# Moving attention blocks between partition quarters: quarters paired 0 with 1 instead of 0 with 2, in another issue order

## The reference

```python
scores = scale * np.matmul(q, k.transpose(0, 1, 3, 2))
thresh = np.max(scores, axis=-1, keepdims=True) - tau
scores = np.where(scores >= thresh, scores, -1000000000.0)
attn = softmax(scores)                      # exp, divided by the sum + 1e-9
x = np.matmul(attn, v)                      # to (2304, 512), heads side by side
h = x @ w_in                                # 512 -> 2048
x = (np.maximum(h, 0.0) + alpha * np.minimum(h, 0.0)) @ w_out
x = ((x @ w1) * (x @ w2)) @ w3 @ w_out2     # 512 -> 1024 -> 1024 -> 512
```

## Time and profile before

| | |
|---|---|
| median of 3 runs | 1023.04 us (1022.2 to 1023.9) |
| the profiled execution | 1022.2 us |
| its span, first to last instruction | 1020.1 us |
| mean granted TensorE clock | 0.987 |
| PE busy / PEld busy / DVE busy | 94% / 85% / 65% of the span |
| DMA moved | 146.95 MB, mean 144 GB/s |
| DMA moves `zbuf<-ybuf` | 256, of which 192 by SP and 64 by ACT |

### The profile page before, as it was taken

One profiled execution on the slowest core, in us unless ns is written; L12 is line 12 of the kernel. 1 busy time (PEld: TensorE's weight loads), 2 busy tenths in 40 slices (PEclk: granted clock), 3 DMA queues, 4 the chain that ended last, 5 costly groups with the idle time before them and its releaser, 6 DMA issues.

```text
span 1020.1 us, 18286 instructions
## 1 busy us (share of the span) xinstructions
PE 959.8 (94%) x6656; PEld 871.2 (85%) x6656; DVE 665.7 (65%) x1648; ACT 417.2 (41%) x976; POOL 514.7 (50%) x604
## 2 busy tenths in 40 slices
PE   3699967999999999999999999999999999999998
PEld 2566635787878787879999999999999999999998
DVE  6899998998999998932333242333765656657544
ACT  5666666666666666533323222222411212103111
POOL 4977878756666766432443333242732524426322
PEclk9799997999999999999999999999999999999999
DMA  7289898776868676657154222222150200200001
GB/s 270 74 256 283 264 323 234 218 211 205 239 188 250 176 217 200 194 158 292 71 191 160 93 94 93 92 94 75 49 207 1 94 1 1 94 1 21 28 1 47
DMA packets 57017, 146.95 MB, mean 144 GB/s; under 512 B 8544, under 2 KB 24928, under 8 KB 54880
## 3 DMA queue, kind: packets, MB, share of 16 engines
q1 hardware_dynamic: 45936, 113.35, 34.5%
q10 hardware_dynamic: 10992, 32.45, 10.9%
HBM read 74.33 MB, written 27.79 MB: 100 GB/s over the span
## 4 chain that ended last, share of the span: by engine, by line
PE 69%; DVE 13%; POOL 5%; issue 4%; DMA 4%; ACT 3%; SPq 1%; ACTq 1%; POOLq 0%
PE psum L843 18%; PE psum L802 11%; PE psum L788 10%; PE psum L855 10%; PE psum L747 9%; PE psum L709 6%; DVE nmx L1107 4%; PE psum L692 3%; DVE e_ring L1120 3%; PE psum L760 2%; DMA zbuf<-ybuf 2%; POOL g L1326 2%; DVE g_raw L1152 1%; DMA k_raw<-k 1%; POOL w_a L1326 1%
## 5 line engine op out<-in xcount | busy, mean ns | idle before, releaser
L1326 POOL TENSOR_TENSOR g<-g_raw,g 128x288 fp32r<-128x288 f32 x160 | 132.7, 840 | 227.5 <-ACT g L982 211.2
L692 PE MATMUL psum<-ks,qs 128*128 128x288 f32 x640 | 119.3, 315 | 39.6 <-DVE e_ring L1120 27.0
L692 PEld LDWEIGHTS psum<-ks,qs 128*128 128x128 f32 x640 | 99.4, 201 | 54.8 <-DVE e_ring L1120 36.7
L1355 POOL TENSOR_SCALAR e_ring<-e_ring,rden,uni 128x576 f32<-128x576 f32 x144 | 119.1, 828 | 53.6 <-DVE rden L1131 47.5
L944 ACT ACTIVATE e_ring<-psum,nmx 128x576 f32<-128x576 f32 x144 | 106.9, 742 | 81.8 <-DVE nmx L1107 81.8
L1152 DVE SCALAR_TENSOR_TENSOR g_raw<-g_raw,beta_sb,psum 128x288 f32<-128x288 f32 x128 | 65.3, 513 | 105.3 <-ACT g_raw L978 105.2
L978 ACT ACTIVATE g_raw<-psum 128x288 f32<-128x288 f32 x128 | 52.6, 411 | 167.8 <-PE psum L788 159.5
L1107 DVE TENSOR_REDUCE nmx<-psum 128x1 f32<-128x576 f32 x144 | 108.4, 753 | 17.9 <-PE psum L692 17.5
L1120 DVE SCALAR_TENSOR_TENSOR e_ring<-psum,thr,e_ring 128x576 f32<-128x576 f32 x144 | 115.3, 800 | 4.9 <-ACT e_ring L944 4.2
L1139 DVE STREAM_TRANSPOSE ybuf<-e_ring 128x576 f32<-128x576 f32 x144 | 110.6, 768 | 0.8 <-POOL e_ring L1355 0.8
L802 PE MATMUL psum<-g,w_b 128*128 128x288 f32 x768 | 106.0, 296 | 4.5 <-POOL g L1326 4.1
(11 more groups left out here) (86 smaller groups left out, 1410.0 us busy)
## 6 DMA issues: line engine op xcount, KB each, us to landing
zbuf<-ybuf SPq DMA_DIRECT2D x96, 180.0 KB, 3.8
zbuf<-ybuf SPq DMA_DIRECT2D x96, 144.0 KB, 3.9
xy<-xs SPq DMA_DIRECT2D x12, 1152.0 KB, 5.2
raw_a<-weights SPq DMA_DIRECT2D x49, 256.0 KB, 6.5
q_raw<-q ACTq DMA_DIRECT2D x16, 576.0 KB, 6.0
xs<-x_hl SPq DMA_DIRECT2D x32, 288.0 KB, 6.5
k_raw<-k ACTq DMA_DIRECT2D x15, 576.0 KB, 7.3
zbuf<-ybuf ACTq DMA_DIRECT2D x32, 180.0 KB, 4.9
```

Source lines behind the costliest of these rows:

```text
L692: last = mm(dst, qs[:, par, at:at + P], ks[:, par, part, h, cols], start=(m == 0), stop=(m == 2 * len(terms) - 1))
L1326: sub = lambda out_, a, hi: nc.gpsimd.tensor_tensor(out_, a, hi.bitcast(F32), ALU.subtract)
L1355: nc.gpsimd.tensor_scalar(e, e, rden[:, i:i + 1], uni[:, i:i + 1], ALU.mult, ALU.add)\
```

## The change

Group 0 now has source quarters 0 and 1, group 1 has 2 and 3. The rest tile has head 0's 64 rows in quarters 0 and 1 and head 1's in 2 and 3, so its two parts in `qs` are contiguous runs of 64 columns with one run of 128 zero columns between them, one memset for each buffer. The value products read neighbouring places of `zbuf`, and `x_half` writes neighbouring places of `x_hl`. The number and sizes of the moves, who issues them, in which steps, and what they wait for stay. Their order is new:

| | SP, in order of issue | ACT |
|---|---|---|
| before, y = 0 | (0,0) (2,2) (0,1) (2,3) (0,2) (2,0) | (0,3) (2,1) |
| before, y = 1 | (1,0) (3,2) (1,1) (3,3) (1,2) (3,0) | (1,3) (3,1) |
| after, y = 0 | (0,0) (0,1) (1,3) (0,2) (0,3) (1,0) | (1,1) (1,2) |
| after, y = 1 | (2,2) (2,3) (3,1) (2,0) (2,1) (3,2) | (3,3) (3,0) |

```diff
-SP_MOVES = [(0, 0), (1, 2), (0, 1), (1, 3), (0, 2), (1, 0)]
-ACT_MOVES = [(0, 3), (1, 1)]
...
-            return zbuf[:, y:QD:2, kt, at:at + (MAIN + (y == h)) * SQ]
+            return zbuf[:, 2 * y:2 * y + 2, kt, at:at + (MAIN + (y == h)) * SQ]
...
-        def shared_q(par):
-
-            return qs[:, par, 2 * MAIN * P:].rearrange("p (h a z i) -> p h a z i", h=2, a=2, z=2)
...
-            return shared_q(par)[:, h, :, h, :], q_raw[:, h, MAIN * P:].rearrange("p (a i) -> p a i", a=2)
+            at = 2 * MAIN * P + 3 * REST * h
+            return qs[:, par, at:at + REST], q_raw[:, h, MAIN * P:]
...
-            dst = [x_hl[:, par, hl, 0:MAIN * P].rearrange("p (t a i) -> p t a i", t=MAIN, a=QD)[:, :, y:QD:2, :]
+            dst = [x_hl[:, par, hl, 0:MAIN * P].rearrange("p (t a i) -> p t a i", t=MAIN, a=QD)[:, :, 2 * y:2 * y + 2, :]
...
-                for b, c in SP_MOVES:
-                    sp.dma_start(*move(n, y, b, c)).then_inc(s_z[y], 16)
+                for k in range(QD):
+                    dst, src = move(n, 2 * y, (2 * y + k) % QD)
+                    sp.dma_start(dst, src).then_inc(s_z[y], 16)
+                    if k % 2 == 1:
+                        dst, src = move(n, 2 * y + 1, (2 * y + 3 + k // 2) % QD)
+                        sp.dma_start(dst, src).then_inc(s_z[y], 16)
...
-                act.dma_start(*move(n, y, *ACT_MOVES[half])).then_inc(s_z[y], 16)
+                dst, src = move(n, 2 * y + 1, (2 * y + 1 + half) % QD)
+                act.dma_start(dst, src).then_inc(s_z[y], 16)
...
-                for h in range(2):
-                    nc.vector.memset(shared_q(par)[:, h, :, 1 - h, :].bitcast(F32), 0.0)
+                nc.vector.memset(qs[:, par, 2 * MAIN * P + REST:2 * MAIN * P + 3 * REST].bitcast(F32), 0.0)
```

More of the change, by code:

```diff
@@ L440, in lo_part @@
                 return ks[:, n % 2, 1, part, cols], raw[:, cols], hi[:, cols]
-            if low >= 8:
-                return hi[DH:P, :, :], raw[DH:P, :, :], hi[DH:P, :, :]
-            cols = slice(low % 2 * 2 * P, (low % 2 + 1) * 2 * P)
+            cols = slice(low % 2 * 2 * P, (low % 2 + 1) * 2 * P) if low < 8 else slice(0, REST)
             return hi[DH:P, cols], raw[DH:P, cols], hi[DH:P, cols]
@@ L461, in x_piece, with move @@
             return x_rest(n % 2, part // 2) if part % 2 else x_half(n % 2, part // 2)
-        def move(n, y, b, c):
-            a = y + 2 * b
+        def move(n, a, c):
             return (zbuf[c * SQ:(c + 1) * SQ, a, 0:FIRST[c + 1] - FIRST[c], :],
```

## The result

| | before | after |
|---|---|---|
| median (8 runs each, same chip) | 1023.07 us | 1035.96 us |
| lowest to highest | 1022.04 to 1024.78 | 1029.22 to 1039.43 |
| profiled span | 1020.1 us | 1035.7 us |

The ratio is 1.0124, with a 95% interval of 1.0094 to 1.0152: slower by 12.9 us. Run a second time, beside other kernels, it was 1.0107 (1.0065 to 1.0150). The forecast was 1026.1 us in a range of 1021.0 to 1033.0: the right sign, a quarter of the size, and the range misses. The profiled execution of after is one of the longer ones, so its stretches add up to more than the median difference.

What follows compares the result with a forecast made beforehand. PE was taken as the bound, with DMA engines nearly full in pairs 3 and 4. Pairs 0 to 4 2.8, pair 12 0.6, ACT's smaller move -0.3: 3.1 us, from 1023.04 to 1026.1 us, range 1021.0 to 1033.0.

Steps and rivals of the forecast that it cites:

- What bounds the kernel; which waits are tight: PE bounds most pairs, DMA engines nearly full in 3 and 4; ten groups of pairs 0 to 4 have at most 0.31 us.
- The 20 us read from the moves' 2% of the chain: Whole kernel: 2% of 1020.1 us, taken as all the path time the change can reach through the moves.
- Layout and memsets at 0: Copies, memsets, PE's weight loads and value products: the new layout was taken to cost or save 0 us.
- The rate of a burst in one half: SP's six moves of a group: 251 to 207 GB/s, costing 0 to 0.84 us a group; 0.28 us taken.
- In pairs 0 to 2 PE has nothing to hide it.: Pairs 0 to 2: both groups' later landings, 2 x 0.28 = 0.56 us a pair, reach PE in full.
- the rival of the separated queues: Pairs 0 to 4: ACT's second move lands earlier, giving 1020 to 1021 us; chance 0.11 over 2 us faster, 0.03 less.
- In pairs 3 and 4 ... I take it in full: Pairs 3 and 4: DMA engines lack room, delayed weight loads make PE wait; 0.56 us a pair charged in full.
- the signs that I had named for being wrong: Earlier group 0 landings, weight loads of pair 3 or 4 shifting beyond the moves' own time, or a moved low-clock stretch.
- Later pairs, 0.6 us: After pair 4 only pair 12 has no slack, +0.6 us; slack covers pairs 6, 8 and 10.
- My upper end for the sum, 1035.6 us: Whole kernel at 0.84 us a group: 8.4 for pairs 0 to 4, 1.7 and 2.8 later, less 0.3: 12.6 us.

Runs made afterwards that it cites:

- e15: The kernel after, unchanged, measured a second time beside other kernels: 1035.29 us, ratio 1.0107 to before.
- e2: The kernel after with source quarters 1 and 2 exchanged, so that each group reads both halves: 1024.91 us, ratio 1.0012 to before.
- e7: The kernel after with the order of before inside each group: 1029.72 us, ratio 1.0057 to before.
- e10: The kernel after with SP's sources alternating between the group's two quarters and destinations in two runs of three in one half: 1039.73 us, ratio 1.0141 to before.
- e18: The kernel after with half of the key and query loads for pairs 8 to 15 alone: 1034.71 us, ratio 1.0102 to before.
- e5: The kernel before with half of the key and query loads from pair 1 on: 1021.20 us, ratio 0.9961 to before.
- e6: The kernel after with half of the key and query loads from pair 1 on: 1024.37 us, ratio 1.0000 to before.
- e17: The kernel before with half of the key and query loads for pairs 1 to 7: 1020.48 us, ratio 0.9962 to before.

## Why the prediction was wrong

*What bounds the kernel; which waits are tight.* Held: PE, and pairs 3 and 4 near-full. That the ten groups of pairs 0 to 4 land just ahead of PE was read rightly, but PE did not wait longer at each of them: in pair 2 it waited 0.59 us before and not at all after. The 20 us read from the moves' 2% of the chain were no bound, since a chain can grow: after, its page gives the moves 4% and SP's issuing of them (L526) another 4%. Groups with slack before became waits: group 1 of pairs 6, 10 and 12, pair 14 besides, pair 8 not; in e15 it is pairs 8, 10, 12 and 14. Two of them, after:

```profile
233.49 0.20 PEld L702 LDWEIGHTS psum<-zbuf,vs 128*64 128x64 f32 x4 [0.71 <-DMA zbuf<-ybuf]
...
396.93 0.20 PEld L702 LDWEIGHTS psum<-zbuf,vs 128*64 128x64 f32 x4 [1.44 <-DMA zbuf<-ybuf]
```

*Layout and memsets at 0.* Held: e2 and e7, and the durations at equal clock.

*The rate of a burst in one half.* The bounds, 251 and 207 GB/s, held; the choice of a third between them was too small. The burst ran at 219 GB/s: 995/219 = 4.54 us for six moves, 0.57 us more than 3.97, where I took 0.28. The Trainium skill, in SBUF — State Buffer, section "Door 1: The DMA port swizzle", gives about 218 GB/s for one half of the partitions, and this case's traces agree, with 213 to 222 in the first burst of the twelve kernels that read one half. The same page, section "Can I just issue two DMAs to hit both halves?", has only 6% for two DMAs on different halves over a single one. That is not quite this case, and a queue of alternating moves gains more here: 255 against 219 GB/s is 16%. I took a small value because in pairs 0 to 4 packets of loads stand between those of the moves. By e2, e7 and e10 that reasoning has no support: amid the loads even the order within a half costs time, and the rate of the lone burst does not give the kernel's time at all.

*"In pairs 0 to 2 PE has nothing to hide it."* 1.7 us of the sum. In the two profiles of after these pairs cost 0.3 and -0.3 us, and in the three others with the same code 1.7, 3.1 and over 4 us, a mean of about 1.8. The size was about right and the steady delay for each group is not what happens: it comes in some executions and not in others. In the first profile group 0 of pair 1 even landed at 80.2, 2.4 us ahead of PE. That fits the rival of the separated queues, for ACT's second move; it could not pay, since PE waits little there anyway.

*"In pairs 3 and 4 ... I take it in full", 1.1 us.* This is the step that failed. The term measured 9.7 us in the profiled execution, 5.4 in e15 and 7.6 in e18. I had written that the DMA engines have no room there and that the moves would push the weight loads PE waits for, but priced it as the moves' own delay, once; even at the measured 0.57 us a group that is 2.3 us. The trace shows the delay carried on: the moves, then ten weight loads of 256 KB issued 2.4 us later and slower to land by 2.1 us, ACT's in-order wait for a weight piece (7.9 against 2.7 us), then pair 4's moves issued 5.7 us late and PE's wait for them (5.7 against 1.9 us). e5 and e6 show that with 8% fewer bytes most of the extra goes. Which link of this multiplies it is not shown, since e2 has nearly the same wait on the weights and no loss. Of the signs that I had named for being wrong, two came: the weight loads shift by more than the moves' own time, and the low clock moves (30.6 us at 1.2 GHz instead of 13.7). What the clock costs is unresolved.

*Later pairs, 0.6 us.* Mis-sized: 4.3 us. With 0.57 instead of 0.28 us a group my own method gives pair 12 1.1, pair 8 0.6, pairs 6 and 10 0.3 each, together 2.3 us. By SP's first moves all of the 4.3 us lie in these four pairs: 0.9, 0.7, 1.1 and 1.5 us in 6, 8, 10 and 12. The places were right; 6, 10 and 12 cost more than the method gives.

My upper end for the sum, 1035.6 us, hit the median by luck: it charges 5.0 us to pairs 0 to 2 and 3.4 to pairs 3 and 4, which took 0.3 and 9.7 in the profiled execution.

## What to carry to other kernels

Let copies between partition quarters read from both halves of the partitions (0 to 63, 64 to 127) in turn; here that is worth some 6 us. If reads must stay in one half, the order of the destinations is worth as much again (e7 against e10); with reads from both halves the new order cost nothing that could be measured (e2). Look at where the DMA share is above 0.9 before pricing a slower transfer: its extra time can be paid by whatever stands behind it in the queue. In pairs 3 and 4 an extra 2.3 us of moves came out as 5 to 10 us; with 8% fewer bytes to move, the whole loss was a quarter. And a lone burst is a poor stand-in for the same copies amid other traffic: by e2 its rate does not give the price.

## What the runs showed of the hardware

In the first 4.6 us of pair 15's moves (144 to 180 KB each), sources that alternate between the halves gave 245 to 255 GB/s in seven kernels, two from one half and one from the other in turn 230 (e2), and sources in one half 213 to 222 in twelve, at DMA shares of 0.88 to 1.07. The order of destinations did not change the rate of a lone burst (214 against 218 GB/s) and changed the kernel by 8 to 10 us amid other traffic (e7 against e10), which I had not expected and can't explain from these profiles. A stretch of 49 us in which the DMA engines were nearly full (0.92 and 0.94) took the same time with about 10 us more of it at 1.2 GHz (e17 against e5).
